# Five of the six weight regions of a two-expert kernel moved by 32 to 224 bytes within a partition

## The chip, the cores and the metric

One NeuronCore of a Trainium2 chip runs the whole kernel as one program. The metric is the device time of one execution in microseconds (us); lower is better.

## What is computed

Attention through 32 "packed" queries per head, then two feed-forward experts over 4608 tokens of width 512, all in float32:

```
p_packed = softmax_attention(p, k, v)            # 32 rows per head
x = softmax_attention(q, p_packed, p_packed)     # 8 x 576 = 4608 tokens, 512 wide
x = rms_norm(x) * rms_g
x = (silu(x @ w_gate) * (x @ w_val)) @ w_out     # first expert, 512 -> 1536 -> 512
h = x @ w_in                                     # second expert, 512 -> 2048
out = (max(h, 0) + alpha * min(h, 0)) @ w_out2   # 2048 -> 512
```

## The kernel before

**Two stages.** Stage 1 does attention and the first expert, in 16 tiles of 288 tokens. Stage 2 does the second expert, in 9 tiles (NT) of 512 tokens. Stage 2 is what the change is about. It begins when stage 1 has ended and fills the second half of the run.

**Three passes.** For nearly float32 accuracy every product is made of three matmuls on fp32r parts (`three_passes`, lines 568 to 570): weights' high part with activations' high part (L568), weights' low part with activations' high part (L569), weights' high part with activations' low part (L570). So each matmul has its own load of 128x128 weights (LDWEIGHTS), and the stream on TensorE is load, matmul, load, matmul throughout. The weight load of a matmul runs while the matmul before it is streaming its activations.

**Stage 2.** For one token tile n, `up(n, f)` makes hidden block f (of 16): 4 slices k of the input width, three passes each, 12 matmuls of 128x512. `down2(n, d)` multiplies the activated hidden block d, again 12 matmuls of 128x512, into 4 output banks. `down2` trails `up` by three blocks. One tile is 16 x 24 = 384 matmuls, nine tiles are 3456. VectorE, ScalarE and GpSimd prepare the operands beside them: VectorE applies the leaky function (L1225, L1228) and takes the low part (L1232), ScalarE makes the high part (L985), GpSimd splits the next token tile `xs` (L548, L550).

**Where the operands lie.** All tiles are placed by hand by `place`, which gives each an address within a partition. The weights of the second expert stand in six regions that overlay tiles of stage 1 that are no longer needed: `w2_hi_front` and `w2_lo_front` hold f = 0 to 9, `w2_hi_mid` and `w2_lo_mid` f = 10 to 13, `w2_hi_back` and `w2_lo_back` f = 14 and 15. One f takes 4096 bytes in its region, and one weight load reads 512 bytes of that. The transferred weights (`w2_raw_*`) lie in the low regions; GpSimd writes the high part into the high region (L542) and the low part over the raw one (L544). The activations of stage 2 are `xs` (two slots, each with a high and a low half of 8192 bytes; a matmul reads 2048 bytes) and `h2_hi`, `h2_lo` (two slots of 2048 bytes).

Before `m_at`, the kernel pads its cursor with

```
        same_rows = 256
        cursor[0] += (gv_at - cursor[0]) % same_rows
```

so that `m_at` has the same remainder by 256 as `gv_at`. All sizes from there on that matter are multiples of 256 bytes, so in stage 2 all six weight regions, `xs`, `h2_hi` and `h2_lo` have one common remainder by 256. The start of every weight slice is a multiple of 512 bytes from its region's start, and that of every activation slice a multiple of 2048 bytes.

**Stage 1** has the same three passes, with 288 columns. Its weights (`m_hi`, `m_lo`, `ow_hi`, `ow_lo`) have that same remainder, but not all of its activations do: `an_hi` and `an_lo` consist of pieces of 4 x 288 = 1152 bytes, and `h_hi` and `h_lo` have three slots (SLOTS) of 1152 bytes each, used in turn by hidden block d as slot d % 3. 1152 is 4.5 times 256. Counted from `an_at`, `h_hi` starts at 12,672 bytes (49.5 times 256) and `h_lo` at 16,128 (63 times 256). So slots 0, 1, 2 of `h_hi` are 128, 0, 128 bytes off the weights' remainder, and those of `h_lo` 0, 128, 0. A hidden block's `down` is 12 matmuls in a row, four times L568, L569, L570.

Of the kernel before, what the change touches and what calls it, by code (L numbers as in the profile page):

```python
# [34 lines left out]
W2_FRONT, W2_MID = 10, 4  # L35
# [59 lines left out]
def build(nc, q_t, k_t, v_s, p_t, w1_gv, w1_o, w2, rms_g, alpha, out_t):  # L95
# [3 lines left out]
    with ExitStack() as ctx:  # L99

        base = -(-nc.sbuf_base // 32) * 32
        cursor = [base]

        def place(name, shape, dt=F32, at=None):

            size = 4
            for n in shape[1:]:
                size *= n
            offset = cursor[0] if at is None else at
            if at is None:  # L110
                cursor[0] += -(-size // 32) * 32
            assert offset + size <= nc.sbuf_usable_end, (name, offset + size - nc.sbuf_usable_end)
            return nc.alloc_sbuf_tensor_at(name, shape, dt, offset=offset)
# [10 lines left out]
        gv_at = cursor[0]  # L124
# [31 lines left out]
        m_at = cursor[0]  # L156
        m_hi = place("m_hi", [P, NF1, GROUPS, GV], F32R)
        m_lo_at = cursor[0]
        m_lo = place("m_lo", [P, NF1, GROUPS, GV], F32R)
        m_raw = place("m_raw", [P, NF1, GROUPS, GV], F32, at=m_lo_at)  # L160
        ow_at = cursor[0]
        ow_hi = place("ow_hi", [P, NF1, MODEL], F32R)
        ow_lo = place("ow_lo", [P, NF1, MODEL], F32R)
# [5 lines left out]
        mean_0 = place("mean_0", [P, 2, HALF], at=q0_at + 4 * PAIRS * SEQ + 2 * step)  # L169
        e2_0 = place("e2_0", [P, 2, GROUPS, HALF], at=q0_at + 4 * PAIRS * SEQ + 4 * step)  # L170
        assert 4 * PAIRS * SEQ + 8 * step <= 4 * 9 * MODEL
        an_at = cursor[0]
        an_hi = place("an_hi", [P, 2, GROUPS, HALF], F32R)
        an_lo = place("an_lo", [P, 2, GROUPS, HALF], F32R)
# [6 lines left out]

        w2_size = 4 * W2_COLS
        xs_size = 2 * 4 * KC * TILE
        assert 2 * W2_FRONT * w2_size <= m_at - gv_at
        assert xs_size + 2 * W2_MID * w2_size <= ow_at - m_at
        w2_back = NF2 - W2_FRONT - W2_MID
        h_size = 4 * 4 * 2 * TILE
        assert xs_size + 2 * w2_back * w2_size + h_size <= an_at - ow_at
        front_lo, mid_at, mid_lo = gv_at + W2_FRONT * w2_size, m_at + xs_size, m_at + xs_size + W2_MID * w2_size
        back_at, back_lo = ow_at + xs_size, ow_at + xs_size + w2_back * w2_size  # L190
        w2_hi_front = place("w2_hi_front", [P, W2_FRONT, W2_COLS], F32R, at=gv_at)
        w2_lo_front = place("w2_lo_front", [P, W2_FRONT, W2_COLS], F32R, at=front_lo)
        w2_raw_front = place("w2_raw_front", [P, W2_FRONT, W2_COLS], F32, at=front_lo)
# [6 lines left out]
        xs_gap = (ow_at - m_at) // 4  # L200
        xs = place("xs", [P, 2, xs_gap], F32R, at=m_at)
        xs_raw = place("xs_raw", [P, 2, xs_gap], F32, at=m_at)
        h2_at = back_at + 2 * w2_back * w2_size
        h2_hi = place("h2_hi", [P, 2, TILE], F32R, at=h2_at)
        h2_lo = place("h2_lo", [P, 2, TILE], F32R, at=h2_at + h_size // 4)
        act2_sb = place("act2_sb", [P, 2, TILE], at=h2_at + h_size // 2)
# [1063 lines left out]
```

## Time and profile before

| | |
|---|---|
| time, median of 3 runs | 1564.51 us (1562.2 to 1564.56) |
| the profiled execution: its own time | 1564.24 us |
| the profiled execution: span | 1562.4 us |
| TensorE (PE) busy | 1549.3 us, 99% of the span |
| weight loads (PEld) busy, beside PE | 1322.4 us, 85% |
| VectorE, ScalarE, GpSimd busy | 749.4, 447.0, 183.4 us |
| granted TensorE clock, mean | 0.999 of full speed |

The span is the profiled execution from its first to its last instruction; its own time is 1.84 us more. In the views, PE is the matmul part of TensorE and PEld its weight loads. A matmul's duration contains its way through the array, so matmuls in a row overlap; what a matmul costs is the distance from its start to the start of the next.

### The profile page before, as it was taken

What the parts mean: (1) busy time and instruction counts of PE and PEld (TensorE: products, weight loads), DVE (VectorE), ACT (ScalarE), POOL (GpSimd) and SP (SyncE); (2) the same over time, 40 slices, a digit from 0 to 9 for tenths busy, and PEclk for the clock granted to TensorE, in tenths of its full rate; (3) what the DMA queues carried; (4) which work ended last, traced back from release to release, by engine and by line L of the source; (5) the groups of instructions that cost most, each with busy time, mean ns of one, the idle gap of its engine ahead of it and who ended that gap; (6) DMA issues with size and microseconds to landing.
All of it is one profiled execution on the core that took longest, in us unless ns stands there. A gap on an engine that the chain in (4) does not pass through costs nothing.

```text
span 1562.4 us, 25626 instructions
## 1 busy us (share of the span) xinstructions
PE 1549.3 (99%) x10326; PEld 1322.4 (85%) x10326; DVE 749.4 (48%) x1279; ACT 447.0 (29%) x849; POOL 183.4 (12%) x132
## 2 busy tenths in 40 slices
PE   8999999999999999999999999999999999999998
PEld 3889889899898989889988888888888888888887
DVE  5765554646555455554543434343443434343333
ACT  4445344444534445342211111111111111111111
POOL 2700000000000000007460001010101001010000
PEclk9999999999999999999999999999999999999999
DMA  9302112021210302003300001010100001010000
GB/s 352 105 20 79 47 40 70 16 79 46 79 47 1 108 17 77 17 17 150 135 16 27 27 0 54 0 54 0 41 13 27 27 10 44 0 54 0 27 0 27
DMA packets 42737, 76.15 MB, mean 49 GB/s; under 512 B 2208, under 2 KB 19616, under 8 KB 42656
## 3 DMA queue, kind: packets, MB, share of 16 engines
q1 hardware_dynamic: 37472, 65.55, 12.3%
q10 hardware_dynamic: 5184, 9.44, 1.5%
q8 instruction: 61, 1.00, 0.3%
q14 instruction: 20, 0.16, 0.0%
HBM read 56.11 MB, written 18.87 MB: 48 GB/s over the span
## 4 chain that ended last, share of the span: by engine, by line
PE 95%; DVE 2%; DMA 1%; ACT 1%; issue 1%; SPq 0%; ACTq 0%; DVEq 0%
PE psum L568 30%; PE psum L569 29%; PE psum L570 29%; PE psum L700 3%; DMA gv_sb<-w_gv 1%; PE psum L662 1%; PE psum L602 1%; PE psum L588 0%; PE psum L650 0%; PE psum L669 0%; PE psum L617 0%; DVE h_lo L1199 0%; DVE act_sb L1196 0%; ACT h_hi L958 0%; ACT o_sb L994 0%
## 5 line engine op out<-in xcount | busy, mean ns | idle before, releaser
L1232 DVE TENSOR_TENSOR h_lo<-g,h_hi 128x512 fp32r<-128x512 f32 x144 | 126.2, 876 | 451.5 <-ACT h_hi L985 451.5
L985 ACT CAST h_hi<-g 128x512 fp32r<-128x512 f32 x144 | 89.4, 621 | 637.2 <-PE psum L570 566.2
L568 PE MATMUL psum<-an_hi,m_hi 128*128 128x288 f32 x768 | 236.5, 308 | 1.2 <-DVE act_sb L1196 0.6
L568 PE MATMUL psum<-h_hi,ow_hi 128*128 128x288 f32 x768 | 233.9, 305 | 0.6 <-DVE h_lo L1199 0.6
L569 PE MATMUL psum<-h_hi,ow_lo 128*128 128x288 f32 x768 | 227.1, 296 | 0.0
L569 PE MATMUL psum<-an_hi,m_lo 128*128 128x288 f32 x768 | 226.7, 295 | 0.0
L570 PE MATMUL psum<-h_lo,ow_hi 128*128 128x288 f32 x768 | 226.2, 295 | 0.0
L570 PE MATMUL psum<-an_lo,m_hi 128*128 128x288 f32 x768 | 225.9, 294 | 0.0
L568 PEld LDWEIGHTS psum<-h_hi,ow_hi 128*128 128x128 f32 x768 | 144.1, 188 | 34.7 <-issue 34.0
L1196 DVE TENSOR_TENSOR act_sb<-act_sb,psum 128x288 f32<-128x288 f32 x192 | 85.9, 448 | 162.4 <-PE psum L570 144.5
L568 PEld LDWEIGHTS psum<-an_hi,m_hi 128*128 128x128 f32 x768 | 144.1, 188 | 22.1 <-issue 16.9
L1199 DVE TENSOR_TENSOR h_lo<-act_sb,h_hi 128x288 fp32r<-128x288 f32 x192 | 109.2, 569 | 107.4 <-ACT h_hi L958 107.4
L569 PEld LDWEIGHTS psum<-an_hi,m_lo 128*128 128x128 f32 x768 | 144.4, 188 | 1.1
L569 PEld LDWEIGHTS psum<-h_hi,ow_lo 128*128 128x128 f32 x768 | 144.6, 188 | 0.1
L570 PEld LDWEIGHTS psum<-h_lo,ow_hi 128*128 128x128 f32 x768 | 144.4, 188 | 0.0
L570 PEld LDWEIGHTS psum<-an_lo,m_hi 128*128 128x128 f32 x768 | 144.3, 188 | 0.0
L568 PE MATMUL psum<-xs,w_hi_front 128*128 (+1 forms) x360 | 140.1, 389 | 0.5 <-ACT y_sb L968 0.5
L568 PE MATMUL psum<-h_hi,w_hi_front 128*128 128x512 f32 x360 | 140.7, 391 | 0.0
L570 PE MATMUL psum<-h_lo,w_hi_front 128*128 128x512 f32 x360 | 140.1, 389 | 0.0
L569 PE MATMUL psum<-h_hi,w_lo_front 128*128 128x512 f32 x360 | 140.1, 389 | 0.0
L569 PE MATMUL psum<-xs,w_lo_front 128*128 (+1 forms) x360 | 140.0, 389 | 0.0
L570 PE MATMUL psum<-xs,w_hi_front 128*128 (+1 forms) x360 | 140.0, 389 | 0.0
(139 smaller groups left out, 2377.1 us busy)
## 6 DMA issues: line engine op xcount, KB each, us to landing
k_sb<-k_t SPq DMA_DIRECT2D x16, 576.0 KB, 5.0
q_sb<-q_t SPq DMA_DIRECT2D x8, 1152.0 KB, 5.9
y_mid<-y_sb SPq DMA_DIRECT2D x16, 576.0 KB, 3.5
xs_raw<-y_mid SPq DMA_DIRECT2D x9, 1024.0 KB, 5.2
out_t<-o_sb ACTq DMA_DIRECT2D x36, 256.0 KB, 2.0
v_sb<-v_s SPq DMA_DIRECT2D x8, 1024.0 KB, 6.5
gv_sb<-w_gv SPq DMA_DIRECT2D x4, 1536.0 KB, 19.3
w_raw_front<-w SPq DMA_DIRECT2D x2, 2560.0 KB, 11.9
```

The source lines that it names most:

```text
L568: nc.tensor.matmul(dst, w_hi, hi, start=start, stop=False)
L569: nc.tensor.matmul(dst, w_lo, hi, start=False, stop=False)
L570: return nc.tensor.matmul(dst, w_hi, lo, start=False, stop=stop)
L602: mm = nc.tensor.transpose(at_ps(c, t)[:, at:at + P], a_sb[:, g, KEY_STARTS[j]:KEY_STARTS[j] + P], ident[:])
L662: mm = nc.tensor.matmul(psum[:, gram_bank(c, h) + e, 0:HALF], gram_sb[:, e, :], a2[:, h, e, :], start=True, stop=True)
L700: mm = nc.tensor.matmul(psum[keys, m_bank(c, j) + e, :].rearrange("p (f n) -> p f n", f=2), pp_tg[dims, pair, :], gv_sb[dims, 2 * j:2 * j ...
L985: nc.scalar.copy(h2_hi[:, f % 2, :], g32[:, f % 2, :]).then_inc(g_hi_done, 1)
L1196: nc.vector.tensor_tensor(act_sb[:, s, :], act_sb[:, s, :], val_ps, ALU.mult).then_inc(h32_done, 1)
L1199: nc.vector.tensor_tensor(h_lo[:, s, :], act_sb[:, s, :], h_hi[:, s, :].bitcast(F32), ALU.subtract).then_inc(h_lo_done, 1)
L1232: nc.vector.tensor_tensor(h2_lo[:, s, :], g32[:, s, :], h2_hi[:, s, :].bitcast(F32), ALU.subtract).then_inc(g_lo_done, 1)
```

## The change

It moves starting addresses and nothing else: no instruction is added, removed or resized. With `apart` = 32 bytes, and counted from the common remainder by 256 of the activations, the regions come to stand at

| region | bytes off before | bytes off after |
|---|---|---|
| `w2_hi_front` | 0 | 0 |
| `w2_hi_mid` | 0 | 32 |
| `w2_lo_front` | 0 | 64 |
| `w2_lo_mid` | 0 | 96 |
| `w2_hi_back` | 0 | 160 |
| `w2_lo_back` | 0 | 224 |

To make room the cursor is advanced by 256 bytes twice: before `ow_at`, which moves `ow_hi` and `ow_lo` and the second slot of `xs`, and before `an_at`, which moves all of stage 1's activations and `y_sb` (512 bytes in all). `h2_at` keeps its remainder.

```
+        apart = 32
+        cursor[0] += 8 * apart
         ow_at = cursor[0]
...
+        cursor[0] += 8 * apart
         an_at = cursor[0]
...
-        front_lo, mid_at, mid_lo = gv_at + W2_FRONT * w2_size, m_at + xs_size, m_at + xs_size + W2_MID * w2_size
-        back_at, back_lo = ow_at + xs_size, ow_at + xs_size + w2_back * w2_size
+        front_lo = gv_at + W2_FRONT * w2_size + 2 * apart
+        mid_at, mid_lo = m_at + xs_size + apart, m_at + xs_size + W2_MID * w2_size + 3 * apart
+        back_at, back_lo = ow_at + xs_size + 5 * apart, ow_at + xs_size + w2_back * w2_size + 7 * apart
...
-        h2_at = back_at + 2 * w2_back * w2_size
+        h2_at = ow_at + xs_size + 2 * w2_back * w2_size + 8 * apart
```

The assertions on the sizes are widened to match.

## Rows read from the trace of the kernel before

**Rows 1.** The page: span, busy time, granted clock, and the chain that ended last

```profile
span 1562.4 us, 25626 instructions
PE 1549.3 (99%) x10326; PEld 1322.4 (85%) x10326; DVE 749.4 (48%) x1279; ACT 447.0 (29%) x849; POOL 183.4 (12%) x132
PEclk9999999999999999999999999999999999999999
PE 95%; DVE 2%; DMA 1%; ACT 1%; issue 1%; SPq 0%; ACTq 0%; DVEq 0%
```

**Rows 2.** Busy time by window, two stretches of stage 2

```profile
core 0: us, PE busy (x) PEld busy (x) DVE busy (x) ACT busy (x) POOL busy (x), PEclk, DMA share, GB/s
900.00:1000.00 100.00, 100.00 (x443) 82.64 (x442) 40.15 (x54) 13.53 (x22) 6.49 (x2) 1.00 0.06 21
1400.00:1500.00 100.00, 100.00 (x443) 82.75 (x442) 37.62 (x56) 13.52 (x22) 0.00 (x0) 1.00 0.03 11
```

**Rows 3.** All waits from 775 to 1555 us that name PE or PEld

```profile
engine line waited for: us in total, times, longest us
ACT h_hi L985 <- PE psum L570: 566.2, 118, 5.4
ACT o_sb L994 <- PE psum L570: 24.0, 16, 2.7
DVE act_sb L1225 <- PE psum L570: 3.8, 1, 3.8
PEld psum L568 <- issue: 1.7, 7, 0.3
```

**Rows 4.** Timeline of PE: stage 2's first two matmuls and its last

```profile
start us, us, engine line op out<-in xcount [idle before <-releaser]
773.66 0.47 PE L568 MATMUL psum<-xs,w_hi_front 128*128 128x512 f32 x1 [0.54 <-ACT y_sb L968]
773.97 0.39 PE L569 MATMUL psum<-xs,w_lo_front 128*128 128x512 f32 x1
...
1557.75 0.39 PE L570 MATMUL psum<-h_lo,w_hi_back 128*128 128x512 f32 x1
```

**Rows 5.** Weight loads in groups, 775 to 1555 us: busy, mean | idle before

```profile
L570 PEld LDWEIGHTS psum<-h_lo,w_hi_front 128*128 128x128 f32 x360 | 67.6, 188 | 14.2
L569 PEld LDWEIGHTS psum<-h_hi,w_lo_front 128*128 128x128 f32 x360 | 67.6, 188 | 13.8
L568 PEld LDWEIGHTS psum<-h_hi,w_hi_mid 128*128 128x128 f32 x144 | 27.0, 188 | 5.6
L569 PEld LDWEIGHTS psum<-xs,w_lo_mid 128*128 128x128 f32 x144 | 27.0, 188 | 5.6
L568 PEld LDWEIGHTS psum<-xs,w_hi_back 128*128 128x128 f32 x72 | 13.5, 188 | 2.8
L569 PEld LDWEIGHTS psum<-xs,w_lo_back 128*128 128x128 f32 x72 | 13.5, 188 | 2.8
```

**Rows 6.** Timeline of PE, stage 1, first and twelfth matmul of `down`: d 5, d 9

```profile
299.95 0.29 PE L568 MATMUL psum<-h_hi,ow_hi 128*128 128x288 f32 x1
...
301.42 0.29 PE L570 MATMUL psum<-h_lo,ow_hi 128*128 128x288 f32 x1
...
315.14 0.29 PE L568 MATMUL psum<-h_hi,ow_hi 128*128 128x288 f32 x1
...
316.61 0.29 PE L570 MATMUL psum<-h_lo,ow_hi 128*128 128x288 f32 x1
```

**Rows 7.** The same for d 4 and d 7, with their ninth and tenth matmul

```profile
295.53 0.29 PE L568 MATMUL psum<-h_hi,ow_hi 128*128 128x288 f32 x1
...
296.59 0.31 PE L570 MATMUL psum<-h_lo,ow_hi 128*128 128x288 f32 x1
296.74 0.30 PE L568 MATMUL psum<-h_hi,ow_hi 128*128 128x288 f32 x1
...
297.01 0.29 PE L570 MATMUL psum<-h_lo,ow_hi 128*128 128x288 f32 x1
...
307.53 0.30 PE L568 MATMUL psum<-h_hi,ow_hi 128*128 128x288 f32 x1
...
308.60 0.31 PE L570 MATMUL psum<-h_lo,ow_hi 128*128 128x288 f32 x1
308.75 0.30 PE L568 MATMUL psum<-h_hi,ow_hi 128*128 128x288 f32 x1
...
309.02 0.29 PE L570 MATMUL psum<-h_lo,ow_hi 128*128 128x288 f32 x1
```

**Rows 8.** Tile w_hi_mid and w_hi_back: first weight load, and GpSimd's last split

```profile
L568 PEld LDWEIGHTS psum<-xs,w_hi_mid x144: 187/188/188, 819.8 to 1535.3; 128*128 128x128 f32 x144
L544 POOL TENSOR_TENSOR w_lo_mid<-w_raw_mid,w_hi_mid x4: 2394/2398/2727, 777.2 to 788.5; 128x1024 fp32r<-128x1024 f32 x4
...
L568 PEld LDWEIGHTS psum<-xs,w_hi_back x72: 187/188/188, 841.5 to 1546.2; 128*128 128x128 f32 x72
L544 POOL TENSOR_TENSOR w_lo_back<-w_raw_back,w_hi_back x2: 2396/2398/2400, 792.3 to 796.3; 128x1024 fp32r<-128x1024 f32 x2
```

**Rows 9.** Tile w_raw_front: GpSimd's low parts, first and last start

```profile
L544 POOL TENSOR_TENSOR w_lo_front<-w_raw_front,w_hi_front x10: 2391/2402/2603, 712.6 to 745.8; 128x1024 fp32r<-128x1024 f32 x10
```

More of the change, by code:

```diff
@@ L183, in build @@
         xs_size = 2 * 4 * KC * TILE
-        assert 2 * W2_FRONT * w2_size <= m_at - gv_at
-        assert xs_size + 2 * W2_MID * w2_size <= ow_at - m_at
+        assert 2 * W2_FRONT * w2_size + 2 * apart <= m_at - gv_at
+        assert xs_size + 2 * W2_MID * w2_size + 3 * apart <= ow_at - m_at
         w2_back = NF2 - W2_FRONT - W2_MID
         h_size = 4 * 4 * 2 * TILE
-        assert xs_size + 2 * w2_back * w2_size + h_size <= an_at - ow_at
-        front_lo, mid_at, mid_lo = gv_at + W2_FRONT * w2_size, m_at + xs_size, m_at + xs_size + W2_MID * w2_size
-        back_at, back_lo = ow_at + xs_size, ow_at + xs_size + w2_back * w2_size
+        assert xs_size + 2 * w2_back * w2_size + h_size + 8 * apart <= an_at - ow_at
+        front_lo = gv_at + W2_FRONT * w2_size + 2 * apart
+        mid_at, mid_lo = m_at + xs_size + apart, m_at + xs_size + W2_MID * w2_size + 3 * apart
+        back_at, back_lo = ow_at + xs_size + 5 * apart, ow_at + xs_size + w2_back * w2_size + 7 * apart
         w2_hi_front = place("w2_hi_front", [P, W2_FRONT, W2_COLS], F32R, at=gv_at)
```

## The prediction

> **What bounds the kernel now.** I read the page first. PE is busy for 99% of the span, its clock is granted in full in every slice, and 95% of the chain that ended last is PE [rows 1]. So the question is what a matmul costs, not who waits for whom. The change concerns stage 2, so I looked there next. In each of the 100 us windows PE has no idle time at the full clock (1.00, the 2.4 GHz level) [rows 2], and among the waits between 775 and 1555 us none is PE's: the other engines wait for PE, and PEld loses 1.7 us in all [rows 3]. Stage 2 is therefore a plain sum: number of matmuls by distance from start to start.
>
> That distance comes from the timeline. From stage 2's second matmul at 773.97 us to its last at 1557.75 us [rows 4] lie 783.78 us and 3454 steps (3456 matmuls, the first left out because it starts cold behind a wait): 226.9 ns each. 512 columns at 2.4 GHz are 213.3 ns. The excess, 13.6 ns a matmul or 47 us in the whole stage, is the only thing on the path that the position of operands could touch. The weight loads tell the same by region: busy plus idle before, divided by the count, is 227.2 ns for `w2_hi_front` under `h_lo`, 226.1 for `w2_lo_front` under `h_hi`, 226.4 in both mid groups and 226.4 in both back groups [rows 5]. All six regions behave alike today, and each load takes 188 ns, 39 ns less than the step that it is hidden in.
>
> **The change part by part.** No instruction is added or taken away, so every cost is a change in the duration or the overlap of what is there.
>
> *Moved weight loads.* Of a hidden block's 24 loads in a tile, 16 read the high region and 8 the low one. In nine tiles that gives 1440 loads from `w2_hi_front`, which stays at 0, and as moved ones 720 (low front, 64 bytes), 576 and 288 (mid, 32 and 96), 288 and 144 (back, 160 and 224): 2016 moved loads of 3456. Each runs while some activation streams, which keeps its remainder. What it costs that the two now start at different remainders, no row of stage 2 shows, since there all are alike. The nearest rows are in stage 1, where the weights have one remainder and the activations alternate between it and 128 bytes off it.
>
> In `down` with slots 0 and 2 the eight matmuls that stream `h_hi` are 128 bytes off and the four that stream `h_lo` are at 0. Slot 2 (d 5) takes 1.47 us from its first start to its twelfth, slot 0 (d 9) also 1.47 us [rows 6]: 11 steps of 133.6 ns. 288 columns at 2.4 GHz are 120.0 ns, so the excess is 13.6 ns. That is what stage 2 shows with every operand at 0. An excess that is the same for 288 and for 512 columns, and the same for mostly 128 off and for all at 0, looks like a fixed cost of changing weights, not like two streams that meet in memory.
>
> In slot 1 it is the other way round: `h_hi` at 0, `h_lo` 128 off. There the same 11 steps take 1.48 us (d 4) and 1.49 us (d 7), and in both blocks one step behind an `h_lo` matmul, the ninth, is 0.15 us instead of 0.13 [rows 7]. So position is not wholly without effect: 135.0 ns on average against 133.6, or +1.4 ns a matmul. The last digit of the rows is worth 0.9 ns of this.
>
> For the moved loads this gives the bounds. Above: if each of the 2016 paid what the worst single step pays (150 less 133.6 = 16.4 ns), 33 us. Below: if each lost the whole excess, 2016 x 13.6 ns = 27.4 us gained. I take 0: the rows nearest in kind (most of the steps 128 off, no idle, full clock) are slots 0 and 2, and they give 0, with the rows' last digit good for 0.9 ns or 1.8 us either way.
>
> Here the Trainium skill speaks against that value. The measured gap between matmuls 13.6 ns above the columns' time [rows 4] is more than the page "TensorE: Matmul & The Clock Gate" allows in its section "Back-to-back issue gap": the columns at 2.4 GHz plus 2.5 ns, about 216 ns for 512 columns. By that figure 11.1 ns a matmul are avoidable, and if separate remainders avoided them for the moved loads, an estimate from that page is 22 us gained, 1542 us. The page measures bf16, and no run here shows that type.
>
> *Stage 1.* `ow_hi` and `ow_lo` move by 256 bytes, the activations by 512 in all. By 256 every remainder stays. By 512 the two weight tensors swap halves against the activations; but slots 0 and 2 of `h_hi` lie 384 and 128 bytes off by 512, and both take 1.47 us [rows 6]. So 0; at one last digit (0.9 ns) over `down`'s 16 x 12 x 12 = 2304 matmuls it is 2.1 us at most, either way.
>
> *GpSimd's splits and the transfers of the weights.* They read and write the moved regions. What hides them is slack: the last mid split starts at 788.5 us and takes 2.7 us, its first use is at 819.8; the last back split starts at 796.3 and takes 2.4, its first use is at 841.5 [rows 8]. The front regions are done by 748.4 us (745.8 and 2.6) [rows 9], 25 us ahead of the stage's start. Were the cover gone, GpSimd's 16 splits would stand in front of TensorE, but the smallest margin is 25 us and nothing here could stretch them so far. Cost 0.
>
> Sum: 1564.24 us, the profiled execution (span 1562.4 and 1.84 around it), plus 0. The runs' median is 0.27 us above that execution, so the forecast is 1564.5 us. About 0.2%, 3.1 us, is what a measurement of this kernel can tell from no change; the likeliest case's own range is 1561 to 1568 us.
>
> **The rivals.**
> *Slower: a load at another remainder collides with the stream.* Place: the steps in which a moved region is loaded. For it speaks slot 1 against slots 0 and 2, the same work on the same engines with only the addresses different [rows 6, 7]; against it, that slots 0 and 2 are 128 bytes off in most steps without paying. Price: at slot 1's mean of 1.4 ns, 2.8 us; at 16.4 ns for one moved load in three (672), 11.0 us. In the middle some 7 us: 1571.5 us. It decides from 1.5 ns per moved load (3.1 us over 2016).
> *Faster: today's common remainder is what costs the 13.6 ns.* For it: the excess is there in every step, the load starts within a few ns of the stream, and both at the same remainder. Against it: slots 0 and 2, whose excess is no smaller [rows 6]. Price: all of it 27.4 us, 1537 us; half of it 13.7 us, 1550.8 us.
> *The change does not do what it says:* the memory distinguishes addresses by a unit in which 32 to 224 bytes are nothing. Then each step stays at 226.9 ns: 1564.5 us, like the forecast. The Trainium skill's page "SBUF — State Buffer", section "Who interferes with whom", would have it so: the moving operand and the weight load have a read port each and wait for nobody. Of two ports nothing is to be seen here; that all loads last 188 ns at every remainder agrees [rows 5].
>
> **How the numbers follow.** No change, with the third rival: 0.46, for the equal excess in both stages. Slower by over 0.2%: 0.36, since slot 1 is the one difference by address that the trace shows, and it is a loss. Faster by over 0.2%: 0.18, since no row shows an excess below 13.6 ns tied to a position. The range goes down to 1555 us (4.7 ns gained per moved load), which leaves out about 0.11 of the faster case, and up to 1577 us (6.2 ns lost per moved load), which leaves out 0.08 of the slower one.
>
> **What the new profile would show.** If the forecast holds: stage 2 again 783.8 us from its second matmul to its last, and busy plus idle of the weight loads at 226 to 227 ns in each region. If positions count, the groups of weight loads by region differ: `w2_hi_front` at 0 stays near 227 ns and serves as the measure, the others stand above or below it, and a cost by distance would order them 32, 64, 96, 160, 224. A lengthened load (over 188 ns) would name the load as the loser, a longer step at 188 ns the stream. The prediction is wrong if 128 bytes, the only distance that the trace shows, is an exceptional one, so that 32, 64 or 96 behave otherwise; or if 512 columns meet the load in another way than 288 do.

## The result and the profile after

The changed kernel takes 1580.01 us (median, 1577.72 to 1582.07), beside 1564.0 us before (four runs each). The ratio is 1.0106, with a 95% interval of 1.0093 to 1.0118: 1.06% slower, some 16 us. It was forecast at 1564.5 us within 1555 to 1577. The slower rival had been given 0.36.

The page of the kernel after, to be held against [rows 1]:

```profile
span 1577.9 us, 25626 instructions
PE 1565.2 (99%) x10326; PEld 1322.5 (84%) x10326; DVE 747.6 (47%) x1279; ACT 446.9 (28%) x849; POOL 183.8 (12%) x132
PEclk9999999999999999999999999999999999999999
```

The counts and the granted clock are the same. The weight loads are as busy as they were (1322.5 us; 1322.4 before). The matmuls are busy for 15.9 us longer, while PE's share of the span stays at 99%. So PE does not wait more, it gets through its stream more slowly. The timeline of PE gives the place, in the matmuls that answer to [rows 4]:

```profile
773.28 0.47 PE L572 MATMUL psum<-xs,w_hi_front 128*128 128x512 f32 x1 [0.53 <-ACT y_sb L972]
773.59 0.39 PE L573 MATMUL psum<-xs,w_lo_front 128*128 128x512 f32 x1
...
1573.28 0.40 PE L574 MATMUL psum<-h_lo,w_hi_back 128*128 128x512 f32 x1
```

(The lines are numbered four higher than before: L572 to L574 are the three passes.) Stage 2 starts at 773.28 us, 0.4 us earlier than before, so stage 1 has no part in it. From its second matmul to its last are 799.69 us, against 783.78: 15.9 us more, all of the loss. Over 3454 steps that is 231.5 ns against 226.9.

The weight loads by group, 775 to 1555 us, answer to [rows 5] (busy, mean of one | idle before). The first line is the kernel before's, of a group that [rows 5] leaves out; the others are the kernel after's:

```profile
L568 PEld LDWEIGHTS psum<-h_hi,w_hi_front 128*128 128x128 f32 x360 | 67.6, 188 | 15.5 <-issue 1.7
...
L574 PEld LDWEIGHTS psum<-h_lo,w_hi_front 128*128 128x128 f32 x360 | 67.7, 188 | 15.2
L573 PEld LDWEIGHTS psum<-h_hi,w_lo_front 128*128 128x128 f32 x360 | 67.6, 188 | 14.6
L572 PEld LDWEIGHTS psum<-h_hi,w_hi_front 128*128 128x128 f32 x360 | 67.6, 188 | 17.6 <-issue 0.2
L572 PEld LDWEIGHTS psum<-xs,w_hi_mid 128*128 128x128 f32 x144 | 27.0, 188 | 6.1
L573 PEld LDWEIGHTS psum<-xs,w_lo_mid 128*128 128x128 f32 x144 | 27.0, 188 | 6.5
```

Two things are to be seen. Every load still lasts 188 ns: the load is not what became longer, only the idle time ahead of it did (6.1 to 6.5 us in 144 mid loads instead of 5.6). And the loads from `w2_hi_front`, which were not moved, are among the dear ones: busy plus idle divided by 360 is 236.7 ns for L572 and 230.3 for L574, where it was 230.8 and 227.2 before. One block of `down2` with front weights shows it as steps:

```profile
1001.84 0.40 PE L572 MATMUL psum<-h_hi,w_hi_front 128*128 128x512 f32 x1
1002.07 0.39 PE L573 MATMUL psum<-h_hi,w_lo_front 128*128 128x512 f32 x1
...
1003.23 0.39 PE L572 MATMUL psum<-h_hi,w_hi_front 128*128 128x512 f32 x1
```

Six steps take 1.39 us, 231.7 ns each.

By region, from start to start in the timeline, the mean steps after are 231.5 ns in front, 231.8 in mid and 231.2 in back. Before they were 226.8, 226.7 and 226.7. The extra is 10.1 us over front's 2160 steps, 4.5 over mid's 864 and 1.9 over back's 432, 16.5 in all. (Steps over 260 ns are left out of these means. The kernel before had eight, which explains the 0.6 us that these sums are above 15.9.) Only 720 of front's 2160 loads had moved, yet its steps cost what those of mid and back do, where all had.

### The profile page after: what moved, and what is told of

Same layout as the page of the kernel before. It is cut to its first block, busy times and chain, and to the rows that moved or that the text cites. A ratio compares the mean times of both kernels' runs of the same rounds, so it can differ in the third digit from the quotient of the medians.

```text
span 1577.9 us, 25626 instructions
## 1 busy us (share of the span) xinstructions
PE 1565.2 (99%) x10326; PEld 1322.5 (84%) x10326; DVE 747.6 (47%) x1279; ACT 446.9 (28%) x849; POOL 183.8 (12%) x132
## 4 chain that ended last, share of the span: by engine, by line
PE 96%; DVE 2%; DMA 1%; ACT 1%; issue 1%; SPq 0%; ACTq 0%; DVEq 0%
PE psum L572 30%; PE psum L573 29%; PE psum L574 29%; PE psum L704 3%; DMA gv_sb<-w_gv 1%; PE psum L666 1%; PE psum L606 0%; PE psum L592 0%; PE psum L654 0%; PE psum L673 0%; PE psum L621 0%; DVE h_lo L1203 0%; DVE act_sb L1200 0%; ACT h_hi L962 0%; ACT o_sb L998 0%
## 5 line engine op out<-in xcount | busy, mean ns | idle before, releaser
L572 PE MATMUL psum<-an_hi,m_hi 128*128 128x288 f32 x768 | 236.5, 308 | 1.3 <-DVE act_sb L1200 0.7
L572 PE MATMUL psum<-h_hi,ow_hi 128*128 128x288 f32 x768 | 233.9, 305 | 0.5 <-DVE h_lo L1203 0.5
L573 PE MATMUL psum<-an_hi,m_lo 128*128 128x288 f32 x768 | 226.7, 295 | 0.0
L574 PE MATMUL psum<-h_lo,ow_hi 128*128 128x288 f32 x768 | 226.2, 295 | 0.0
L574 PE MATMUL psum<-an_lo,m_hi 128*128 128x288 f32 x768 | 226.0, 294 | 0.0
L572 PEld LDWEIGHTS psum<-h_hi,ow_hi 128*128 128x128 f32 x768 | 144.1, 188 | 34.7 <-issue 34.0
L572 PEld LDWEIGHTS psum<-an_hi,m_hi 128*128 128x128 f32 x768 | 144.1, 188 | 22.2 <-issue 17.1
L574 PEld LDWEIGHTS psum<-h_lo,ow_hi 128*128 128x128 f32 x768 | 144.5, 188 | 0.0
L574 PEld LDWEIGHTS psum<-an_lo,m_hi 128*128 128x128 f32 x768 | 144.3, 188 | 0.0
L572 PE MATMUL psum<-xs,w_hi_front 128*128 (+1 forms) x360 | 141.5, 393 | 0.5 <-ACT y_sb L972 0.5
L572 PE MATMUL psum<-h_hi,w_hi_front 128*128 128x512 f32 x360 | 141.4, 393 | 0.0
L574 PE MATMUL psum<-xs,w_hi_front 128*128 (+1 forms) x360 | 140.6, 391 | 0.0
L574 PE MATMUL psum<-h_lo,w_hi_front 128*128 128x512 f32 x360 | 140.5, 390 | 0.0
```

Source lines behind the costliest of these rows:

```text
L572: nc.tensor.matmul(dst, w_hi, hi, start=start, stop=False)
L573: nc.tensor.matmul(dst, w_lo, hi, start=False, stop=False)
L574: return nc.tensor.matmul(dst, w_hi, lo, start=False, stop=stop)
```

## Experiments

All of them start from the kernel before, and give each region an offset through its starting address:

```
+        cursor[0] += ROOM          # ahead of ow_at, and again ahead of an_at
...
+        front_at, front_lo = gv_at + FH, gv_at + W2_FRONT * w2_size + FL
+        mid_at, mid_lo = m_at + xs_size + MH, m_at + xs_size + W2_MID * w2_size + ML
+        back_at, back_lo = ow_at + xs_size + BH, ow_at + xs_size + w2_back * w2_size + BL
```

Since front, mid and back are read in separate blocks, one profile holds three pairs of offsets (high, low). A time given without an interval is that of one execution, and so are all step means. The results together; step means are distances from start to start in the timeline, in ns, steps over 260 left out:

| run | offsets front / mid / back | front | mid | back | time, us |
|---|---|---|---|---|---|
| before | 0,0 / 0,0 / 0,0 | 226.8 | 226.7 | 226.7 | 1564.0 |
| after | 0,64 / 32,96 / 160,224 | 231.5 | 231.8 | 231.2 | 1580.0 |
| e1_room | 0,0 / 0,0 / 0,0 | 226.8 | 226.7 | 226.7 | 1563.9 |
| e2_all64 | 64,64 / 64,64 / 64,64 | 233.3 | 233.3 | 233.3 | 1586.1 |
| e3_128 | 0,128 / 128,128 / 128,256 | 231.3 | 232.7 | 233.7 | 1582.4 |
| e4_32 | 0,32 / 32,32 / 32,256 | 233.3 | 233.4 | 232.3 | 1586.4 |
| e6b_small | 16,16 / 256,256 / 8,8 | 231.3 | 226.8 | 230.8 | 1574.0 |
| e7_far | 192,192 / 160,160 / 224,224 | 229.2 | 233.0 | 233.2 | 1576.3 |
| e16_front | 0,64 / 0,0 / 0,0 | 231.0 | 227.2 | 227.0 | 1573.9 |

**The room alone (e1_room).** ROOM = 256 as in the change, all offsets 0.

> Only the room of the change (256 bytes ahead of ow_at, 256 ahead of an_at); all six weight regions at the activations' remainder as before. Theory A (the offsets of the regions cost the 16 us): 1564 us, every region's step at 226.7 ns. Theory B (the moves by 256 and 512 bytes cost it, which would explain why even loads from the unmoved high front region got slower): 1580 us, steps near 231.5 ns.

1563.88 us, ratio 0.9998 (0.9988 to 1.0007), every region as before. Theory A holds: it is the offsets, and the moves of `ow_at` and `an_at` cost nothing that can be told from noise.

**One common offset (e2_all64).** All six regions 64 bytes off, ROOM = 256.

> All six regions moved by the same 64 bytes; activations not moved. Theory A1 (a load at another remainder than the streaming activations costs): all 3456 loads are moved, not 2016, so at least 1580 us, and some 1591 if the price is per moved load (16 us x 3456/2016 = 27 us). Theory A2 (what costs is that the high and the low region have different remainders, so that a block's loads in turn start at two remainders): they are equal here, so 1564 us.

1586.13 us, ratio 1.0134 (1.0115 to 1.0153). The weight loads, 775 to 1555 us:

```profile
L576 PEld LDWEIGHTS psum<-xs,w_lo_front 128*128 128x128 f32 x360 | 67.7, 188 | 16.3
L577 PEld LDWEIGHTS psum<-xs,w_hi_front 128*128 128x128 f32 x360 | 67.7, 188 | 16.3
L576 PEld LDWEIGHTS psum<-xs,w_lo_mid 128*128 128x128 f32 x140 | 26.3, 188 | 6.3
```

(67.7 + 16.3) / 360 = 233.3 ns, at 188 ns a load, and by the timeline the step is 233.3 ns in all three regions. So at one offset the regions are alike, and they can be compared with each other below. That refutes A2: high and low at one remainder are dear too when it is not the activations'. Of A1 its minimum is met (above 1580 us), but not its price: 3456 moved loads cost 22 us, not 27, so the cost is not a fixed sum per moved load.

**128 and 32 bytes in pairs (e3_128, e4_32).** ROOM = 512.

> Pairs (high, low) of offsets by region: front (0, 128), mid (128, 128), back (128, 0 by 256). Theory A1: a step is dear where the region being loaded is at 128: one step of three in front, all three in mid, two of three in back. Theory A2: all steps of front and back are near 231 ns, mid at 226.7. Theory C (128 bytes is free, as most of stage 1 suggested): all three regions at 226.7, about 1564 us.

> Pairs (high, low) of offsets by region: front (0, 32), mid (32, 32), back (32, 0 by 256). Theory A1: mean step of front +1/3, mid in full, back 2/3 of the price of a moved load (7.9 ns at 16 us over 2016 loads): 229.3, 234.6 and 231.9 ns. Theory A2: front and back near 231.3, mid at 226.7.

Mid at (128, 128) takes 232.7 ns a step, so theory C falls: 128 bytes is not free in stage 2. A2 falls once more in both. A1's proportion falls too: in front with (0, 32) one load of three is off and the step is 233.3 ns, as dear as mid with all three off (233.4), where A1 had 229.3. So the price does not count the loads that are off: one region off can cost a block as much as both, and at 128 bytes two loads of three off (back of e3_128, 233.7 ns) cost more than all three (mid, 232.7).

**Only the low front region (e16_front).** This is the front part of the change by itself, ROOM = 512.

> Only the low front region at 64; the rest at 0. If the price is that of a block in which any load is off: front at 231.5 ns in all three passes taken together (2160 steps x 4.8 ns, 10 us: 1574 us), mid and back 226.7. If only the moved load pays, 720 x 6.7 ns: 1569 us. If the disturbance carries over into later blocks, mid and back are above 226.7 too.

1573.86 us, ratio 1.0064 (1.0045 to 1.0082). Loads, 775 to 1555 us:

```profile
L577 PEld LDWEIGHTS psum<-h_lo,w_hi_front 128*128 128x128 f32 x360 | 67.7, 188 | 14.8
L576 PEld LDWEIGHTS psum<-h_hi,w_lo_front 128*128 128x128 f32 x360 | 67.6, 188 | 14.3
L575 PEld LDWEIGHTS psum<-h_hi,w_hi_front 128*128 128x128 f32 x360 | 67.6, 188 | 18.0 <-issue 1.4
L576 PEld LDWEIGHTS psum<-xs,w_lo_mid 128*128 128x128 f32 x144 | 27.0, 188 | 5.7
L577 PEld LDWEIGHTS psum<-xs,w_hi_mid 128*128 128x128 f32 x144 | 27.0, 188 | 5.8
```

The first of the three theories holds: 720 moved loads make all 2160 front steps dearer (231.0 ns on average, 9 us; with both regions at 64 it was 233.3 ns). Within the three passes the step in which L576's matmul streams is the longest (235.8 ns on average in the timeline; L575's 228.9, L577's 228.4), and during it an unmoved high weight is loaded. Which step is the longest depends on the distance: in front of e4_32 (0, 32) it is L575's with 239.0 ns, during which the moved low weight is loaded, beside 228.6 for L576 and 232.2 for L577. In both runs all three passes are above 226.7. Mid and back stay within 0.5 ns of their old step, so little carries over.

**The finest unit and the period (e6b_small), and the far side (e7_far).** ROOM = 512. For 16 and 8 bytes the tensors of front and back are four and two elements longer and read from there on.

> Both weight regions of each group moved alike: front by 16 bytes, mid by 256, back by 8. If the period is 256 bytes, mid is at 226.7 ns. If 16 bytes is the finest unit of the memory, back (8 bytes) is at 226.7 and front (16 bytes) dear, near 233; if the unit is 32 bytes, both are at 226.7.

> Both weight regions of each group moved alike: front by 192 bytes, mid by 160, back by 224. If any distance but 0 by 256 costs the same, all three are at 233.3 ns like the shared 32 and 64 bytes, 1586 us. If the cost is a curve in the distance with 128 slightly cheaper (232.7), 160 lies near 232.7 and 224 near 233.3.

Mid at 256 bytes is back at 226.8 ns, so the period of 256 bytes is confirmed. But 8 bytes cost 4.1 ns and 16 bytes 4.5: neither 16 nor 32 bytes is the unit, and both branches of that expectation fall. Nor is the cost one sum for every distance, or a smooth curve in it: 192 bytes is the cheapest (229.2), 160 and 224 are at 233.0 and 233.2, and 8 bytes already costs three fifths of the worst (4.1 of 6.7 ns).

**Which relation counts (e5b_follow, e9_base).** ROOM = 512. In the first `h2_hi` and `h2_lo` are moved by 64 bytes and the mid weights with them; in the second everything from `gv_at` on.

> h2_hi and h2_lo moved by 64 bytes together with the mid weights; xs, front and back weights stay at 0. Relative theory (what counts is the load's remainder against the streaming activations): up is cheap with front and back (226.7 ns) and dear with mid (233.3 ns), down is dear with front and back and cheap with mid. Absolute theory (a weight region not at the old place costs by itself): up and down of mid are dear, up and down of front and back cheap.

> All operands of stage 2 (and most tiles of stage 1), weights and activations, moved together by 64 bytes; all relations kept. If only the relation of the addresses counts: 226.7 ns a step, 1564 us. If the absolute address counts: 233.3 ns, 1586 us.

e9_base took 1563.85 us with 226.8, 226.7 and 226.7 ns: for a common move by 64 bytes only the relations count, the absolute address does not. e5b_follow took 1576.26 us and is inconclusive. By block, `up` is at 229.9 (front), 233.1 (mid) and 227.6 ns (back), `down` at 230.9, 230.1 and 230.2. Mid's `down` and front's `up`, where load and stream have one remainder and which the relative theory had at 226.7, are dear too. Neither theory covers that. It suggests that it does not suffice for a matmul's own operands to agree when those of the blocks around it don't; but here `xs` and `h2` also differ from each other, which no run tried by itself.

**Does stage 1 pay, and why so little (e8_stage1, e10_w288, e10_w448, e14_w448_same, e15_w448_64).** In e8_stage1 `ow_hi` and `ow_lo` are 64 bytes off and stage 2 is left alone. In the others every matmul of stage 2 streams only a part of its columns:

```
-  hidden_ps(f % 4), ... x_hi_of(n % 2)[:, k, :], x_lo_of(n % 2)[:, k, :]
+  hidden_ps(f % 4)[:, 0:W], ... x_hi_of(n % 2)[:, k, 0:W], x_lo_of(n % 2)[:, k, 0:W]
```

with the same for `down2`, and one short matmul per output bank at the start of the program. The output columns beyond W are left out. e10 has the offsets 0,0 / 64,64 / 128,128, e14 all 0, e15 all 64; ROOM = 512 throughout.

> Stage 2 as before; in stage 1 ow_hi and ow_lo are moved by 64 bytes, so that in down no load is at the remainder of its activations (64 or 192 bytes off). If the cost per step of stage 2 (6.7 ns) holds for 288 columns too, 2304 matmuls cost 15 us more and 11 steps of a down block take 1.54 us instead of 1.46; if stage 1's 128 bytes already pay it in part or 288 columns are immune, little changes: 1564 us.

> Every matmul of stage 2 streams only the first 288 of its 512 columns (the other 224 columns of the output are left out); both weight regions of front at 0, of mid at 64, of back at 128 bytes. If the width is what makes stage 1 immune: all three groups at 133.3 ns a step (120.0 and 13.3). If it is something else of stage 1: front near 133.3, mid and back 6 ns above.

> The same with 448 columns (the other 64 left out). 448 columns are 186.7 ns. If wide matmuls pay: front 200.0, mid and back 206 ns a step. If only 512 columns (2048 bytes) pay, all at 200.0.

> 448 of 512 columns in stage 2 (64 left out), all six regions at the activations' remainder. If a common remainder is cheap at this width too: 200.0 ns a step everywhere. If only 512 columns have the cheap state: 202 to 204 ns as in the run with mixed offsets.

> The same with all six regions 64 bytes off. If 448 columns behave like 512: 206.7 ns a step. If the offset does not matter at this width: the same as with all at 0.

e8_stage1: 1564.13 us. In the timeline of PE its `down` blocks d 4 and d 9, first and twelfth matmul, answer to [rows 6, 7]:

```profile
295.58 0.29 PE L577 MATMUL psum<-h_hi,ow_hi 128*128 128x288 f32 x1
...
297.04 0.29 PE L579 MATMUL psum<-h_lo,ow_hi 128*128 128x288 f32 x1
...
315.16 0.30 PE L577 MATMUL psum<-h_hi,ow_hi 128*128 128x288 f32 x1
...
316.61 0.29 PE L579 MATMUL psum<-h_lo,ow_hi 128*128 128x288 f32 x1
```

1.46 and 1.45 us for 11 steps, where they were 1.48 and 1.47: no load of `down` is at its activations' remainder any more, and it does not cost the 6.7 ns a step. Over all steps of `down` below 170 ns the timeline gives 132.4, 132.5 and 132.5 ns for slots 0, 1 and 2, where it gave 132.3, 133.9 and 132.5 before. What a common remainder in all slots gives is seen in e13_slots5 below.

e10_w288, a mid block (64 bytes off) of stage 2:

```profile
925.68 0.29 PE L575 MATMUL psum<-xs,w_hi_mid 128*128 x1
...
927.14 0.29 PE L577 MATMUL psum<-xs,w_hi_mid 128*128 x1
```

1.46 us for 11 steps, 132.7 ns each, as in stage 1. Over all steps below 260 ns mid (64) is at 133.6 ns, back (128) at 133.6 and front (0) at 136.3. But front's mean is not that of its position. With so few columns PE outruns the other engines, it waits for ScalarE and VectorE at tile changes (16 waits, 21.6 us), and behind such a wait (1.80 us at 903.52 us) the granted clock is at its lower level, 1.2 GHz:

```profile
904.40:907.60 3.20, 3.20 (x16) 3.20 (x15) 2.05 (x3) 1.05 (x2) 0.00 (x0) 0.50 0.18 68
```

That is a window of 3.20 us in which PE is busy throughout; the 0.50 is the granted clock, and a step is 240 ns there. Of the steps between 150 and 260 ns 99 fall into front, which begins a tile, and 7 into mid and back. Over the steps below 150 ns, which leaves these out, front is at 131.7 ns, mid at 133.1 and back at 133.3. So the common remainder is the cheapest here too, but by 1.4 to 1.6 ns and not by 6.0 to 6.7. The narrow width is enough to make position cheap; nothing else of stage 1 is needed.

With 448 columns, 186.7 ns of columns:

```profile
L576 PEld LDWEIGHTS psum<-xs,w_lo_mid 128*128 128x128 f32 x144 | 27.0, 188 | 2.2
L577 PEld LDWEIGHTS psum<-xs,w_hi_mid 128*128 128x128 f32 x144 | 27.0, 188 | 2.3
```

That is e14_w448_same, all at 0: 203.6 ns a step in all regions by the timeline, at 1495.34 us. The same loads of e15_w448_64:

```profile
L576 PEld LDWEIGHTS psum<-xs,w_lo_mid 128*128 128x128 f32 x144 | 27.0, 187 | 2.2
L577 PEld LDWEIGHTS psum<-xs,w_hi_mid 128*128 128x128 f32 x144 | 27.0, 187 | 2.2
```

202.2 ns a step, at 1490.44 us. (e10_w448 with mixed offsets: 202.8, 202.0 and 204.0, at 1492.09 us.) The expectation of 200.0 ns for a common remainder falls, and so do both values named for e10_w448 and for e15_w448_64: at this width agreement even costs 1.4 ns more than 64 bytes off. At 512 columns a common remainder gives the least step, 13.3 ns above the columns; at 288 columns the mean steps seen lie from 11.7 (front here, at 0) to 14.8 ns above them (slot 1 of stage 1 before); at 448 no region's mean comes below 15.3 ns.

**Stage 1's slots (e12_slots, e13_slots5).** The slots of `act_sb`, `h_hi` and `h_lo` are 1280 bytes apart, ROOM = 0:

```
-        h_hi = place("h_hi", [P, SLOTS, HALF], F32R)
+        h_hi = place("h_hi", [P, SLOTS, 320], F32R)[:, :, 0:HALF]
```

> Only stage 1 changed: slots of act_sb, h_hi and h_lo 1280 instead of 1152 bytes apart, so that all start at the weights' remainder. If slot 1's dearer steps come from its 128 bytes, its down blocks take 1464 ns over 11 steps like the others (about 1 us less in all); if not, they stay at 1469 to 1483 ns. No more than 1 us of 1564 either way.

> Stage 1's slots 1280 bytes apart, as in the run before, now timed: down blocks at 1453 ns per 11 steps instead of 1464 to 1483 save 1 to 3 us: ratio 0.998 to 0.9995, if it can be told from noise at all.

e12_slots took 1561.74 us. Its expectation had two branches, and neither came: not only slot 1 but all three slots went to a median of 1454 ns over 11 steps, from 1465, 1483 and 1464. So slots 0 and 2 had been paying as well, 1.0 ns a step by these medians, and slot 1 2.6 ns (by the mean of all steps below 170 ns it is 0.5 and 0.6, and 2.0). e13_slots5, the same kernel timed, took 1562.45 us, ratio 0.9988 (0.9979 to 0.9997): 0.1% faster than the kernel before, just clear of noise. Its 192 `down` blocks together are 2.2 us shorter, and by that mean the slots are at 131.8, 131.9 and 132.0 ns. In its timeline `down` d 4, slot 1, which answers to [rows 7]:

```profile
294.80 0.30 PE L575 MATMUL psum<-h_hi,ow_hi 128*128 128x288 f32 x1
...
296.26 0.29 PE L577 MATMUL psum<-h_lo,ow_hi 128*128 128x288 f32 x1
...
771.98 0.47 PE L575 MATMUL psum<-xs,w_hi_front 128*128 128x512 f32 x1 [0.54 <-ACT y_sb L975]
```

11 steps take 1.46 us instead of 1.48, and stage 2 starts at 771.98 us instead of 773.66. That start alone would show little: in runs whose stage 1 keeps its relations it lies anywhere from 772.5 (e6b_small) to 775.2 us (e2_all64).

## Why the prediction was wrong

*What bounds the kernel* was right. PE's stream set the time before and after, no wait appeared, and the loss is a longer step in stage 2 and nothing else.

*Which terms are 0* was right for two of three: stage 1 did not move with the 256 and 512 bytes (e1_room), GpSimd's splits and the transfers stayed hidden, and stage 2 started on time.

*The failed step* is "I take 0: the rows nearest in kind ... are slots 0 and 2, and they give 0". They were near in kind in everything but the width. The term "moved weight loads" was 15.9 us, not 0. Stage 1's 288 columns pay little for position: e8_stage1 put all of `down`'s weights off and lost nothing against the kernel before, and in stage 2's own blocks cut to 288 columns (e10_w288) 64 and 128 bytes cost 1.4 and 1.6 ns. At 512 columns the same distance of 128 bytes, in mid of e3_128, cost 6.0 ns a step. Nor did slots 0 and 2 give 0 at their own width. They had been compared with stage 2 at 512 columns; the comparison at 288 columns, which the old trace did not hold, shows them 0.5 to 1.0 ns dearer than a common remainder (e12_slots, e13_slots5). The sentence "the same for 288 and for 512 columns ... looks like a fixed cost of changing weights" read as evidence what was the meeting of two cases: a narrow width that pays some 1 ns for being off, and a wide one at the one common remainder where it is cheap. Two decimals of a microsecond could hardly tell them apart. The prediction had named this way to be wrong (512 columns meeting the load otherwise than 288), without giving it the weight of the range.

*The slower rival* was the right one, but its mechanism was half right. Position costs, and the loads at 188 ns show that the stream is what loses. But it priced moved loads. The upper reach of its middle, 11.0 us, was 672 loads at 16.4 ns. The runs show a price of the block: 2.4 to 6.7 ns on its mean step, by the offsets, once any weight region in it is off, the unmoved loads' steps included. For the change that is 3456 steps at 4.6 ns, 15.9 us. Counted over the 2016 moved loads it would be 7.9 ns each, above the 6.2 at which the range ended; hence the 3 us by which it missed. For the same reason `w2_hi_front` could not serve as the measure that the prediction wanted it to be.

*The faster rival* fell: no offset at 512 columns made the step shorter than 226.7 ns, so the common remainder is not what costs the 13.6 ns. At 448 columns leaving it gained 1.4 ns a step, which the prediction could not know of.

*Slot 1*, the one sign of position in the old trace, was real: with the slots all at one remainder its steps became equal to the others' (e13_slots5). But it was a sign from a mild case: 1.4 ns in the prediction, 2.6 ns against the common remainder, up to 6.7 at 512 columns.

*The third rival*, by which 32 to 224 bytes are nothing, fell: with the same instructions 64 bytes make the step 226.7 or 233.3 ns (e2_all64). The Trainium skill's page "SBUF — State Buffer", section "Who interferes with whom", gives the moving operand and the weight load independent ports and has TensorE wait for nobody; as a rule for timing it is contradicted by these two numbers. Whether the ports are where the two meet, no run shows. The prediction let the loads' 188 ns "at every remainder" speak for that rule, but [rows 5] hold only one remainder. The runs show 187 to 189 ns in the front groups at others (e6b_small), while the step grew by 4.5: the load's duration does not show the cost.

*The avoidable 11.1 ns* were not found. The gap of about 216 ns for 512 columns, which the Trainium skill's page "TensorE: Matmul & The Clock Gate" gives in its section "Back-to-back issue gap" for a matmul in isolation, was not reached by any arrangement tried; the least was 226.7 ns.

*Left open.* What meets what inside the memory was not shown. A load and a stream meeting in one part of the memory would fit the period of 256 bytes and the loads' unchanged 188 ns, but by itself neither the cost of 8 bytes, nor the steps of unmoved loads, nor the 448 columns, which are dearer at 0 than at 64, nor e5b_follow. An arrangement in which the streams keep step from one matmul to the next and which any one offset disturbs would fit those better, and is only argued.

## What to carry to other kernels

In a saturated TensorE stream of 512 columns place the weights and activations at one common remainder by 256 bytes, and keep all regions there: one region off made a whole block of matmuls pay. At another width try it first: at 288 columns the common remainder was worth 0.5 to 2.6 ns a step, at 448 it cost 1.4. Take the price of a placement from rows of the same width. A cost that is equal in two shapes is no proof that it is fixed. In a stage whose only term is steps times distance, a spread of 1 ns between otherwise equal blocks is a reason to widen the range by that term's whole count.

## What was unexpected of the hardware

A matmul's step depends on the relation of operand addresses within a partition: at 512 columns 226.7 ns at a common remainder by 256 bytes; 230.8 at 8 bytes off, 231.3 at 16, 233.4 at 32, 233.3 at 64, 232.7 at 128, 233.0 at 160, 229.2 at 192, 233.2 at 224, and 226.8 again at 256 (weights of both parts moved alike, each distance in one region of one run, 64 in all three). The weight load's own duration is 188 ns in all of the 512-column rows shown. At 288 columns the step is 131.7 ns at 0, 133.1 at 64 and 133.3 at 128 (e10_w288, at the full clock); at 448 it is 203.6 ns at 0 and 202.2 at 64. Moving all operands together by 64 bytes changes nothing.
